# Moving routing steps, the end of attention and the first weight loads in an attention and mixture-of-experts kernel

## What is computed

```python
# q, k, v: (4, 8, 576, 64); window 128
scores = where(0 <= i - j < 128, q @ k.T / 8 - slope[h] * |i - j|, -1e9)
x = softmax(scores) @ v                    # -> rows: (2304, 512)
logits = x @ w_gate                        # (2304, 8)
for idx in argsort(-logits.flatten()):     # greedy: best logit first
    if token unassigned and expert has < 288 tokens: assign
x[tokens of e] = relu(x[tokens of e] @ w1[e]) @ w2[e]    # 512 -> 1024 -> 512
h = x @ w_in                               # 512 -> 2048
out = (h * sigmoid(h)) @ w_out             # 2048 -> 512
```

## Time and profile before

| | us |
|---|---|
| median of 3 runs | 894.51 (893.71 to 894.56) |
| the profiled execution | 896.79 |
| its span, first to last instruction | 895.0 |
| attention and the end of its block | 0 to 194 |
| routing of the first expert, gather | 194 to 226 |
| A 0 to M 7 | 226 to 890 |

### The profile page before, as it was taken

One profiled execution on the slowest core, in us unless ns is written; L12 is line 12 of the kernel. 1 busy time (PEld: TensorE's weight loads), 2 busy tenths in 40 slices (PEclk: granted clock), 3 DMA queues, 4 the chain that ended last, 5 costly groups with the idle time before them and its releaser, 6 DMA issues.

```text
span 895.0 us, 17483 instructions
## 1 busy us (share of the span) xinstructions
PE 846.1 (95%) x6605; PEld 790.2 (88%) x6605; DVE 503.9 (56%) x1618; ACT 344.8 (39%) x814; POOL 290.1 (32%) x306
## 2 busy tenths in 40 slices
PE   6999999962999999999999999999999999999998
PEld 6999999951998998899899889998998899899996
DVE  6667676757667386466628462666376466632111
ACT  4666666621333432433333233333332433433222
POOL 1333233413124422622432244225322522532223
PEclk9999999965899999999999999999999999999999
DMA  6666666414203121230412040403121240312000
GB/s 154 168 153 158 152 154 156 112 28 121 83 13 121 44 76 37 86 107 13 122 44 76 1 121 1 123 9 122 54 65 55 68 114 5 121 60 61 1 1 35
DMA packets 117252, 71.42 MB, mean 80 GB/s; under 512 B 61616, under 2 KB 103600, under 8 KB 117168
## 3 DMA queue, kind: packets, MB, share of 16 engines
q1 hardware_dynamic: 114192, 60.85, 25.2%
q0 software_dynamic: 2976, 9.44, 3.4%
HBM read 60.83 MB, written 9.44 MB: 79 GB/s over the span
## 4 chain that ended last, share of the span: by engine, by line
PE 65%; DVE 10%; DMA 2%; issue 1%; ACT 1%; POOL 1%; SPq 0%; POOLq 0%; DVEq 0%
PE hp L1148 11%; PE hp L1150 10%; PE hp L1149 10%; PE acc L1218 7%; PE acc L1220 7%; PE acc L1219 7%; PE acc L1148 4%; PE acc L1150 3%; PE acc L1149 3%; PE rt L1102 2%; DVE test L1360 2%; DVE h_raw L1561 1%; DMA rows<-x_rows,tokens 1%; DVE wa_l L1498 1%; DMA wa_raw<-in_moe_w_dram 1%
## 5 line engine op out<-in xcount | busy, mean ns | idle before, releaser
L1078 POOL TENSOR_TENSOR h_l<-h_raw,h_h 128x256 fp32r<-128x256 f32 (+1 forms) x128 | 103.6, 809 | 268.2 <-ACT h_h L1315 268.0
L1148 PE MATMUL hp<-xy_h,res_h 128*128 128x256 f32 (+1 forms) x512 | 154.6, 302 | 2.3 <-DVE h_raw L1561 2.3
L1561 DVE TENSOR_TENSOR h_raw<-hp,gate 128x256 f32<-128x256 f32 (+1 forms) x128 | 58.3, 456 | 171.1 <-ACT gate L1307 170.1
L1149 PE MATMUL hp<-xy_l,res_h 128*128 128x256 f32 (+1 forms) x512 | 151.4, 296 | 0.0
L1150 PE MATMUL hp<-xy_h,res_l 128*128 128x256 f32 (+1 forms) x512 | 151.3, 295 | 0.0
L1064 POOL TENSOR_TENSOR wb_l<-wb_raw,wb_h 128x512 fp32r<-128x512 f32 x64 | 86.5, 1353 | 139.6 <-ACT wb_h L1261 139.4
L1307 ACT ACTIVATE gate<-hp 128x256 f32<-128x256 f32 (+1 forms) x128 | 52.4, 409 | 171.0 <-PE hp L1150 170.0
L1218 PE MATMUL acc<-res_h,h_h 128*128 128x512 f32 x288 | 116.7, 405 | 0.0
L1220 PE MATMUL acc<-res_h,h_l 128*128 128x512 f32 x288 | 113.6, 395 | 0.0
L1219 PE MATMUL acc<-res_l,h_h 128*128 128x512 f32 x288 | 113.5, 394 | 0.0
L1148 PEld LDWEIGHTS hp<-xy_h,res_h 128*128 128x128 f32 x512 | 96.6, 189 | 8.5 <-DVE h_raw L1561 4.9
(11 more groups left out here) (214 smaller groups left out, 1754.3 us busy)
## 6 DMA issues: line engine op xcount, KB each, us to landing
wa_raw<-in_moe_w_dram SPq DMA_DIRECT2D x64, 256.0 KB, 2.9
wb_raw<-in_moe_w_dram SPq DMA_DIRECT2D x64, 256.0 KB, 3.1
q_rows<-in_q_dram SPq DMA_DIRECT2D x32, 128.0 KB, 3.8
k_rows<-in_k_dram SPq DMA_DIRECT2D x32, 128.0 KB, 3.0
v_rows<-in_v_dram SPq DMA_DIRECT2D x32, 128.0 KB, 2.4
stage<-in_moe_w_in_dram SPq DMA_DIRECT2D x8, 512.0 KB, 4.5
x_rows<-x_rows_sb SPq DMA_DIRECT2D x16, 256.0 KB, 4.2
stage<-in_moe_w_out_dram SPq DMA_DIRECT2D x8, 512.0 KB, 4.6
```

The lines of the kernel that those rows point to most:

```text
L1078: pool.tensor_tensor(h_l[:, cols], h_raw[:, cols], h_h[:, cols].bitcast(FP32), ALU.subtract).then_inc(g_low, 1)
L1148: nc.tensor.matmul(out_, weights_h, cols_h, start=start, stop=False)
L1149: nc.tensor.matmul(out_, weights_h, cols_l, start=False, stop=False)
L1561: nc.vector.tensor_tensor(h_raw[:, h_cols(s, f)], hp[(A_NO[s, f] - 1) % 2][:, 0:width], gate[:, 0:width], ALU.mult).then_inc(g_done, 1)
```

## The change

It touches five places. (1) In the last pair of attention the first three tiles are transposed before the last weighted values and multiplied by `w_gate` while DVE normalises the rest; the last two tiles follow together; ACT makes both copies. (2) The first expert's comparisons are cut 14 to 6 tiles instead of 10 to 10. (3) The setup moves from slot 3 to slot 2, before `h_l` of a2, and the steps from slots 8, 9, 12, 13, 16, 17, 21, 22, 24, 25, 28, 31, 33 to 7, 8, 11, 12, 16, 20, 24, 25, 27, 28, 31, 34, 38; the gather moves from 31 to 34 with step 11, and the first splits of the next expert's weights from 31, 33, 35, 37 to 34, 36, 38, 40. (4) Of the first expert's weights only wa 0 and wa 1 are loaded before the gather is issued; the others wait for it, and their splits move into the slots of A 0. (5) In the first a tile of each stage all four high-by-high products come first, then the four with low weights, then the four with the low input, each waiting for its own part.

```diff
-LG = P
+def main_tiles(g):
+    return TB - 1 if g + 1 < NG else TB - 2
+def logits_at(g):
+    return P * (TB - main_tiles(g))
...
+            def turn_x_main(g):
                 c = slice(P * (g % PAIRS), P * (g % PAIRS + 1))
                 to = bank("x", g)
-                pe.wait_ge(norm_done, tiles_of_pair(g))
-                for t in range(TB - 1):
+                pe.wait_ge(norm_done, tiles_of_pair(g) if g + 1 < NG else TILES_TO[NS - 2])
+                for t in range(main_tiles(g)):
                     last = nc.tensor.transpose(to[:, P * t:P * (t + 1)], x_rows[:, t, c], ident[:])
                 last.then_inc(turned, 1)
...
+            turn_x_main(NG - 1)
             weighted_values(NS - 1)
-            turn_x(NG - 1)
-            gate_logits(NG - 1)
+            bank("e", NG - 1)
+            gate_logits(NG - 1, slice(0, main_tiles(NG - 1)))
+            turn_x_end(NG - 1)
+            gate_logits(NG - 1, slice(main_tiles(NG - 1), TB))
...
+            copy_x_last(NG - 1)
             copy_x_end(NG - 1)
...
-            copy_x(NG - 1)
             add_logits(NG - 1)
...
-SETUP_AT = {FIRST[2 * _j - 2] + 3: _j for _j in range(1, E)}
-HOOK_LIST = {_j: [FIRST[2 * _j - 2] + _n for _n in (8, 9, 12, 13, 16, 17, 21, 22, 24, 25, 28, 31, 33)]
+SETUP_AT = {FIRST[2 * _j - 2] + 2: _j for _j in range(1, E)}
+HOOK_LIST = {_j: [FIRST[2 * _j - 2] + _n for _n in (7, 8, 11, 12, 16, 20, 24, 25, 27, 28, 31, 34, 38)]
              for _j in range(1, E)}
...
+AHEAD = 14
+SECOND = 672
...
-LOADS = sorted([(kind, w) for w in range(E * FT1) for kind in "ab"], key=lambda load: load_key(*load))
-SPLIT_A, SPLIT_B = {}, {}
+LOADS = sorted([(kind, w) for w in range(RING, E * FT1) for kind in "ab"], key=lambda load: load_key(*load))
+LOADS = [("a", 0), ("a", 1), ("b", 0), ("a", 2), ("b", 1), ("a", 3), ("b", 2), ("b", 3)] + LOADS
+SPLIT_A, SPLIT_B = {0: [3]}, {0: [0], 1: [1], AT[0, "b", 0]: [2], AT[0, "b", 1]: [3]}
...
+                if (kind, w) == LOADS[2]:
+                    sp.wait_ge(fetch_sent, 1)
...
             fetch(0)
             pool.memset(mark[:], 0.0).then_inc(fetch_sent, 1)
-            for w in range(RING):
-                low_b(w)
...
+            def first_tile(out_, weights_h, weights_l, cols, high_ready, low_ready, ready):
+                for c in range(DC):
+                    pe.wait_ge(high_ready, ready + c + 1)
+                    nc.tensor.matmul(out_, weights_h[c], xy_h[:, c, cols], start=(c == 0), stop=False)
+                for c in range(DC):
+                    nc.tensor.matmul(out_, weights_l[c], xy_h[:, c, cols], start=False, stop=False)
+                for c in range(DC):
+                    pe.wait_ge(low_ready, ready + c + 1)
+                    last = nc.tensor.matmul(out_, weights_h[c], xy_l[:, c, cols], start=False, stop=(c == DC - 1))
+                last.then_inc(a_done, 1)
...
-            for w in range(RING):
-                high_a(w)
-                high_b(w)
+            high_a(0)
+            high_a(1)
             for c in range(DC):
                 high_x(0, c, acc[c])
+            high_a(2)
...
             low_a(2)
-            low_a(3)
             after(0, HOOKS[0] - 1)
```

More of the change, by code:

```diff
@@ L550, in copy_x_end, with copy_x_last @@
                     act.wait_ge(lg_done, g)
[L551 removed]
+                w = P * main_tiles(g)
+                nc.scalar.activation(xT[:, w:TB * P], m_ps[n % 2][:, 0:TB * P - w], ACT.Copy).then_inc(e_taken, 1)
+            def copy_x_last(g):
+                n = TURN_NO["x", g]
+                w = P * main_tiles(g)
+                act.wait_ge(turned, n + 1)
+                act.wait_ge(lg_done, g)
+                nc.scalar.activation(xT[:, 0:w], m_ps[n % 2][:, 0:w], ACT.Copy).then_inc(x_taken, 1)
             def exponentials(s):
@@ L898, in experts @@
         at_least = test[:, 0:NT * KW[1]].rearrange("p (t k) -> p t k", k=KW[1])
-        halves = [test[:, o:o + KW[0] * NT // 2].rearrange("p (t k) -> p t k", k=KW[0]) for o in (0, SECOND)]
+        pieces = [test[:, o:o + KW[0] * n].rearrange("p (t k) -> p t k", k=KW[0])
+                  for o, n in ((0, AHEAD), (SECOND, NT - AHEAD))]
         onehot = test[:, 0:NT * BLOCK].rearrange("p (t k) -> p t k", k=BLOCK)
@@ L1092, in part @@
                     pe.wait_ge(half_part, h // 2)
-                    for t in range(NT // 2):
+                    for t in range(AHEAD):
                         nc.tensor.matmul(rt[:, 0:E], test[:, KW[0] * t:KW[0] * t + P], choice[:, t, :],
@@ L1098, in part @@
                 if h < CLOSE[j] and h % 2 == 0:
-                    for t in range(NT // 2 if j == 0 and h > 0 else 0, NT):
-                        o = KW[j] * t if j > 0 or h == 0 else SECOND + KW[0] * (t - NT // 2)
+                    for t in range(AHEAD if j == 0 and h > 0 else 0, NT):
+                        o = KW[j] * t if j > 0 or h == 0 else SECOND + KW[0] * (t - AHEAD)
                         last = nc.tensor.matmul(rt[:, 0:E], thresholds[:, o:o + P], choice[:, t, :],
@@ L1159, in expert_a @@
                 pe.wait_ge(wa_low, w + 1)
+                out_ = hp[(no - 1) % 2][:, 0:CAP]
+                if f == 0:
+                    if i > 0:
+                        pe.wait_ge(x_low, i * DC + 1)
+                    first_tile(out_, [wa_h[w % RING][:, P * c:P * (c + 1)] for c in range(DC)],
+                               [wa_l[w % RING][:, P * c:P * (c + 1)] for c in range(DC)], cols,
+                               x_high, x_low, i * DC)
+                    return
                 for c in range(DC):
-                    if f == 0:
-                        pe.wait_ge(x_low, i * DC + c + 1)
                     m = slice(P * c, P * (c + 1))
-                    last = product(hp[(no - 1) % 2][:, 0:CAP], wa_h[w % RING][:, m], wa_l[w % RING][:, m],
+                    last = product(out_, wa_h[w % RING][:, m], wa_l[w % RING][:, m],
                                    xy_h[:, c, cols], xy_l[:, c, cols], c == 0, c == DC - 1)
@@ L1189, in dense_a @@
                 bank_free(no - 2)
-                for c in range(DC):
-                    if f == 0:
-                        pe.wait_ge(y_low, (STAGES[s - 1][1]) * DC + c + 1)
-                    m = slice(F2 * c + P * f, F2 * c + P * (f + 1))
+                tile = [slice(F2 * c + P * f, F2 * c + P * (f + 1)) for c in range(DC)]
+                if f == 0:
+                    first_tile(hp[(no - 1) % 2][:, 0:width], [res_h[:, m] for m in tile], [res_l[:, m] for m in tile], cols,
+                               y_high, y_low, STAGES[s - 1][1] * DC)
+                    return
+                for c, m in enumerate(tile):
                     last = product(hp[(no - 1) % 2][:, 0:width], res_h[:, m], res_l[:, m],
```

50 lines of the change are left out of this document (28 added, 22 removed).

## The result

The changed kernel takes **908.21 us** (median of 4 runs, 907.45 to 908.85) against 894.53 us for the kernel before in the same comparison (893.71 to 895.84): a ratio of 1.0151, interval 1.0134 to 1.0169. It is slower by 13.7 us, where 2.0 us less were predicted.

A forecast was written before the change was run, and what follows sets the result against it. PE bounds the kernel from 226 us on, with 13.2 us of waits, besides the hand-over chain. Terms -1.6 - 0.25 - 3.7 + 0.85 + 11.8 - 13.2 + 3.5 + 0.6 = -2.0 us give 892.5 us, range 889.0 to 899.0.

The forecast's parts named there:

- The end of attention and the cut of the comparisons: Before the first expert: earlier logits give -1.6 us, and the 14 to 6 cut over five routing rounds -0.25 us.
- The gather in less company: Last gather before A 0: lands in 3.1 us instead of 6.0 with two loads ahead; a1 starts 3.7 us earlier.
- the whole hand-over: From the end of attention to a1 of A 0: first product 5.6 us earlier.
- The setup in A 1 to A 6: Setup ahead of h_l of a2 delays a4 in six stages: +11.8 us in all.
- The new wait at step 8: Six stages M: PE reaches step 8 before DVE's comparison is done, 0.59 us each, +3.5 us.
- The 13.2 us of old waits: Expert stages: PE's waits at step 12 (9.2), for h_raw (3.2) and at step 1 (0.8) go.
- the seven waits of 1.3 us that left it up: Argument against a clock fall at a4: seven earlier PE waits of 1.3 us had left the clock up.
- The third rival: Clock falls at a4's wait in six stages, 2.8 us each, +17 us: 909 us; chance 0.05.
- POOL's splits move into slots where POOL is idle: A 0: the first expert's late weight splits were taken to go into idle POOL slots.
- +0.85 for the setup of A 0: A 0: the setup one slot earlier costs only 0.85 us, since slow tiles give DVE more time.
- POOL's queue behind `h_l` of a10: Stages M: gather and splits end just before PE asks at b11; 0.1 us a stage, +0.6 us in all.
- rival (b): POOL's queue becomes the bound and b11 waits, +1.0 us in six stages: 898.5 us, slower; chance 0.12.

The follow-up runs named there:

- experiment 7: experiment 6 with the first expert's loads and splits as in the kernel before, all eight loads ahead of the gather: 879.25 us, 0.9812 of the kernel before.
- experiment 2: The kernel before with only the setup moved from slot 3 to slot 2: 916.97 us, 1.0241 of the kernel before.
- experiment 4: The changed kernel with POOL's low halves of wb 0 to 2 in slot 0 and wb 3 in slot 1 of A 0: 906.67 us.
- experiment 3: The changed kernel with twelve unread products on PE ahead of a4 of every stage A: 903.47 us, 1.0097 of the kernel before.
- experiment 8: experiment 6 with the early split order of experiment 4, late loads kept: 877.95 us, 0.9802 of the kernel before.
- experiment 1: The changed kernel with the setup back at slot 3, behind h_l of a2: 891.21 us, 0.9957 of the kernel before.
- experiment 5: The changed kernel with the setup and all 13 steps back in their old slots: 893.64 us, 0.9985 of the kernel before.
- experiment 6: The changed kernel with setup at slot 3, steps 0 to 3 one slot later, 6 to 12 one earlier: 880.55 us, 0.9837 of the kernel before.

## Why the prediction was wrong

**Right in place and size.** The end of attention and the cut of the comparisons: -1.85 predicted; the gather's last issue came 2.1 us (experiment 7) and 2.5 us (changed kernel) earlier. The gather in less company: 3.3 us from issue to the transposes, where 3.1 to the landing were taken; the whole hand-over together -5.6 predicted and -6.0 measured, by executions that differ there by up to 1.0 us. The setup in A 1 to A 6: +11.8 predicted, 12.3 measured (1.9 to 2.2 us each). The new wait at step 8: 0.4 us six times, 0.59 with its hidden part, as predicted. The 13.2 us of old waits did go.

**Failed: "against it: the seven waits of 1.3 us that left it up".** The third rival, given 0.05, was what happened in kind. Its argument carried the clock's behaviour from waits of 1.3 us to one of 1.9 us. Behind idle times of 1.7 to 2.4 us before a4 of A 1 to A 6 the clock fell in six stages of six (experiment 2), in three of six (the changed kernel) and in four of six (experiment 4). A fall cost 1.3 to 1.5 us, half of the rival's 2.8, so that the term is +3.9 us in A 2, A 4 and A 6 instead of the rival's 17. The rival's 909 us are close to the result by luck: it was twice too dear for a fall, it had six falls for three, and two other terms failed with it. The Trainium skill, TensorE: Matmul & The Clock Gate, section "What's actually happening", says that activity releases a throttled default state; the runs agree in that more work removed all falls (experiment 3). The prediction had weighed that rule against the earlier trace rows and let the row for a shorter wait decide.

**Failed: "POOL's splits move into slots where POOL is idle", and with it +0.85 for the setup of A 0.** POOL was idle there and DVE was not. The setup took 7.9 us instead of 4.8, a4 waited 4.2 us (4.0 and the 0.15 that each wait hides), and the clock stayed at its lower level for nearly all of the 6.6 us of the window shown above: M 0 started 5.1 us later than predicted. The prediction had the price in hand, 3.04 against 2.12 us for a comparison beside POOL, and applied it to steps 7 and 8, not to the setup that was being moved. The later steps did not meet POOL more often but less: the changed kernel's 21 comparisons on `key_hi` have a median of 2.12, where before had 3.04:

```profile
L1419 DVE SCALAR_TENSOR_TENSOR test<-rungs,base,key_hi x21: 2112/2115/3001, 232.4 to 752.3; 128x1820 bf16<-128x1820 f32 x21
```

Experiments 2, 4 and 8 show the cause: without the low halves beside the setup A 0 loses only the 0.8 us, and with them moved ahead of it the comparison is back at 2.12 us.

**Mis-sized: POOL's queue behind `h_l` of a10, +0.1 a stage.** In M 1 of the changed kernel:

```profile
368.98 1.31 POOL L1106 TENSOR_TENSOR wb_l<-wb_raw,wb_h 128x512 fp32r<-128x512 f32 x1
370.44 1.21 POOL L1084 DMA_INDIRECT rows<-x_rows,tokens  x1
...
373.19 1.24 POOL L1084 DMA_INDIRECT rows<-x_rows,tokens  x1 [0.30 <-issue]
374.44 0.75 POOL L1118 TENSOR_TENSOR h_l<-h_raw,h_h 128x256 fp32r<-128x256 f32 x1
...
375.25 0.50 PE L1279 MATMUL acc<-res_h,h_h 128*128 128x512 f32 x1 [0.47 <-POOL h_l L1118]
```

The gather took 4.0 us instead of the 3.5 of the earlier trace rows, and that half microsecond is what b11 waited for: 2.5 + 6 x 0.15 = 3.4 us in six stages against 0.6. Otherwise the chain was read rightly, but it had only 0.1 us of slack. In M 0 to M 6 the seven gathers took 3.39 to 3.83 us in the kernel before and 3.50 to 4.27 in the changed one. The lengths aren't chance: stage by stage, experiment 1 repeats those of the changed kernel and experiments 5 and 6 those of the kernel before, to 0.02 us. So the length goes with the gather's place; why it is longer behind `h_l` of a10 stays open. It is rival (b) at half its price, by a longer gather and not by a late `h_l` of a10.

**The sum.** A 0 5.1, three falls 3.9, the waits of A 1 to A 6 0.5, b11 2.8: 12.3 of the 13.1 us between -2.0 and +11.1. Part of the other 0.8 is a wait in M 5, 0.5 us with its hidden part, for an `h_raw` that DVE began late:

```profile
717.34 4.82 DVE L1557 TENSOR_TENSOR wa_l<-wa_raw,wa_h 128x512 fp32r<-128x512 f32 x1
...
720.32 1.29 POOL L1106 TENSOR_TENSOR wb_l<-wb_raw,wb_h 128x512 fp32r<-128x512 f32 x1
...
722.75 0.44 PE L1182 MATMUL hp<-ident,rows 96*128 96x96 f32 x3 [0.33 <-DVE h_raw L1619]
```

A low half of wa that takes 0.69 us alone lasted from 717.34 to 722.16, while POOL worked without a break until 721.61. It is the hold-up of A 0 once more, and longer. The rest isn't explained. The remaining 2.6 us of the error in the median come from the kernel before: its profiled execution lay 2.3 us above its median and the changed one's 0.4 below. I shifted by 2.3 as if an execution's excess carried over. About 1 us of it goes with the clock: of 27 executions of the kernel before beside the experiments, ten had a mean granted clock of 0.974 or 0.975 and took 895.7 us in the mean, the others (0.978 or 0.979) 894.6, and the profiled one had 0.975. Why the rest was long isn't settled.

**The range.** It gave the clock 0.05 and had no case in which terms fail together, though each of the three failed terms hangs on DVE or POOL being late. With the clock at a chance of 0.3 the upper end would have had to take in that rival.

## What to carry to other kernels

A wait that is put in front of a busy TensorE has two prices, the idle time and what the clock does behind it; if the idle time is longer than any that the trace shows with the clock up, price a fall for each. Before work is moved into slots where one of DVE and POOL is idle, look at what the other does there: operations of both that run at once can hold each other up, here by 1.7 us for an operation of POOL and by 4.1 us for one of DVE. Where the slack behind a transfer is 0.1 us, its length at the old place is no bound for the new one.

## What the runs showed of the hardware

- The clock mostly fell while PE was busy again: 1.00 in 395.70 to 397.60 of A 2, with PE busy for 0.15 of 1.90 us, 0.81 and 0.50 in the windows behind it. In A 1 to A 6 of the changed kernel and experiments 2 and 4 all 13 falls came 0.5 to 1.5 us after a4's start. In the longest wait, 4.0 us in A 0 of the changed kernel, it fell before PE resumed: 1.00 in 232.30 to 235.30, 0.50 in 235.35 to 236.20, with PE idle in both.
- The same wait in the same place gives a fall in one stage and none in the next: 1.87 us in A 1 left the clock up, 1.82 us in A 2 did not.
- DVE and POOL stretch each other: POOL's low half from 1.3 to 2.97 us beside a comparison of 2.12, DVE's `liked` from 0.32 to 1.43, an operation with one input from 0.17 to 1.26, and a low half of wa from 0.69 to 4.82 beside a run of POOL's operations. The Trainium skill, VectorE: DVE Perf Modes, section "Two Vector instructions with no wait between them", says that the interface shared with GpSimd is read for the second of two SBUF inputs and, in a 2-port mode, for a single one. The first kind agrees; whether L83 runs in such a mode no row here shows.
- The three indirect DMAs of a gather kept POOL for 3.4 to 3.8 us in one kernel and for 3.5 to 4.3 in the other, their issues lasting 0.9 to 1.4 us each, and every stage's length came back to 0.02 us in kernels with the gather at the same place.
